# Routing search in six rounds of 7 and 5 x 5 bits beside the experts, with packed count products

## The chip, the cores and the metric

The kernel runs on one core of a Trainium2 chip. The core has TensorE (PE in the rows; PEld is its weight load), VectorE (DVE), ScalarE (ACT), GpSimd (POOL) and SyncE (SP), which work in parallel, each through its own queue in order, and wait for one another by semaphores. The metric is the time of one execution in microseconds; the profile's times are counted from the span's start.

## The reference

A recurrent attention makes 3072 rows x of 384 numbers, a router with capacity sends each row to one of eight experts, and a shared two-layer network follows:

```python
f = 1.0 / (1.0 + np.exp(-f_logit))
for t in range(S):
    state = f[:, :, t, :, None] * state + np.einsum('bhd,bhe->bhde', k[:, :, t], v[:, :, t])
    y[:, :, t] = np.einsum('bhd,bhde->bhe', q[:, :, t], state)
...
logits = x @ w_gate
for idx in np.argsort(-logits.flatten()):
    tok, e = (int(idx) // E, int(idx) % E)
    if assigned[tok] >= 0 or counts[e] >= cap:        # cap = N // E = 384
        continue
    assigned[tok] = e
    counts[e] += 1
...
h = np.maximum(x[mask] @ w1[e], 0.0)                  # 384 -> 1024
out[mask] = h @ w2[e]                                 # 1024 -> 384
...
h = x @ w_in                                          # 384 -> 2048
g = np.where(h > 0.0, h, np.exp(np.minimum(h, 0.0)) - 1.0)
g @ w_out                                             # 2048 -> 384
```

## The kernel before

**Stages.** `attention` runs to about 135 us of the span. Then `route_and_feed` finds the first expert that fills up and its 384 rows, and from about 174 us it runs eight experts, one after the other, 0 to 7. While TensorE computes expert k, VectorE searches the rows of expert k+1.

**An expert.** Each weight matrix and each activation is split in a high and a low part, and a product is three matmuls: high by high, low weight by high, high weight by low. A block is nine matmuls with 384 columns. The order of blocks on TensorE is written out in `order()`: eight "h" (first layer, `hidden`), each feeding a "y" (second layer, `output`); the last two y blocks are done column by column ("y_end" 0 to 2, `output_end`, six matmuls each); then "g01" (gates 0 and 1 together) and "g" 2 to 15 (`gated`), each followed some blocks later by its "o" (`back`). The last three o blocks of an expert stand between the next expert's first h blocks. ScalarE reads each gate from PSUM (L1177, L1178, L1181) and makes the high part t_hi (L1169), GpSimd makes `whole` (L1109) and the low part t_lo (L1081), and the o block waits for t_lo (L1449). At the end of y, ScalarE copies y_hi (L1193) and VectorE subtracts y_lo (L1522). The last thing in `output_end` is a wait of TensorE for its own last product (`y_done`), after which it raises `used`.

**The search.** For each expert to come, the threshold is found digit by digit. A round is: VectorE computes the limits of all values of the digit (L1588), compares the 24 tiles of `best` with them (L1548; `compare_first`, L100, for the first digit) into `slot_hot`; TensorE counts by products with `held` (a "visit", L1289, or L1285 where two tiles of 64 limits stand side by side in one product and VectorE adds the halves by L1596); VectorE compares the counts with the room (L1597 or L1599); TensorE sums the result (a visit, L1294); VectorE reads the digit (L1601) and adds it to `prefix` (L1607). Digits are 7, 7, 6, 6, 6 bits beside experts (7, 5, 5, 5, 5, 5 for the first search, which runs alone). Four visits follow: sums by `held_over` (L1299, whose input comes by L1613 to L1619), ties (L1301), offsets (L1304) and the list (L1315). `order()` holds a table that says behind which block each visit stands: one for expert 0 (`start`), one for experts 1 to 5, one for expert 6 (`last`). TensorE works in order, so a visit whose input isn't there holds everything behind it. The y_lo of the running expert stand in VectorE's row between two steps of the search (`visits_before_y`).

**Behind the search.** `begin(k + 2)` makes the next `best`, `compare_halves` does the first comparison of the search after next's start (two L100 of 1536 elements), and then VectorE makes w_low of the next expert's weights (L1533), x_lo (L1527) and the rest of w_low (L1539). Ahead of the first w_low it waits for `rows_asked`, which GpSimd raises behind the last of three gathers of the next rows (L1061); these stand in GpSimd's row between its steps on gates 7 to 9 (9 to 11 in expert 0). The gathered rows are turned by TensorE (`turn_x`, L1347) in three steps behind o blocks, all through the same bank r_ps; step m waits for x_lo of step m - 1.

**Expert 0.** GpSimd also makes w_out_low there, two (L1092) behind each t_lo of an h.

## Time and profile before

| | us |
|---|---|
| median of 3 runs | 852.0 (851.53 to 852.79) |
| profiled execution, time | 847.2 |
| its span | 845.5 |
| TensorE busy in the span | 784.0 (93%) |
| VectorE | 497.0 (59%) |
| ScalarE | 465.1 (55%) |
| GpSimd | 524.9 (62%) |

TensorE ends the chain that ended last with 81% of it. A busy share is a mean over stages: the attention to 135 us, the first search to 174 us, and eight experts, of which those from 263.7 us on take 78 to 83 us each. The matmuls are pipelined: a duration of 0.34 us with the next one starting 0.176 us later is TensorE at its full rate, so what an expert loses is read from the starts.

### The profile page before, as it was taken

How to read it: one execution, taken by the hardware profiler on the slowest of the kernel's cores; microseconds unless marked ns; L12 is line 12 of the kernel's file. 1: busy time of each engine (PE TensorE's matmuls, PEld its weight loads, DVE VectorE, ACT ScalarE, POOL GpSimd, SP SyncE). 2: the span in 40 equal slices, each digit the busy share in tenths (PEclk: the TensorE clock that was granted, in tenths of full speed). 3: DMA queues.
4: the chain of work that ended last, by engine and by line, in shares of the span. 5: the costliest groups of instructions: out<-in, count | busy, mean ns of one | idle time of the engine just before them, and what ended most of it. 6: DMA issues, size and time to landing. Idle time of an engine off the chain costs nothing.

```text
span 845.5 us, 17776 instructions
## 1 busy us (share of the span) xinstructions
PE 784.0 (93%) x6078; PEld 743.5 (88%) x6078; DVE 497.0 (59%) x1035; ACT 465.1 (55%) x980; POOL 524.9 (62%) x500
## 2 busy tenths in 40 slices
PE   3999995488989999999999999999999999999995
PEld 2888884487989999999999999999999999999995
DVE  6899988884695567457645863586457516430001
ACT  5677766141674277427742864287337734753653
POOL 8788883467775368537852775287518754954552
PEclk9999997598999999999999999999999999999998
DMA  6777691400130041004100410040004004100000
GB/s 195 209 210 208 191 366 45 174 14 1 60 115 6 29 150 29 2 28 150 29 5 26 151 29 16 14 160 19 29 2 159 20 29 150 29 1 29 2 1 29
DMA packets 33740, 65.70 MB, mean 78 GB/s; under 512 B 4560, under 2 KB 20944, under 8 KB 33280
## 3 DMA queue, kind: packets, MB, share of 16 engines
q1 hardware_dynamic: 27072, 50.36, 18.1%
q0 software_dynamic: 3136, 9.64, 3.5%
q10 hardware_dynamic: 3456, 4.72, 1.6%
q8 instruction: 44, 0.72, 0.3%
q14 instruction: 32, 0.26, 0.1%
HBM read 55.26 MB, written 9.44 MB: 77 GB/s over the span
## 4 chain that ended last, share of the span: by engine, by line
PE 81%; POOL 6%; issue 4%; DVE 3%; ACT 3%; DMA 2%; SPq 0%; ACTq 0%; POOLq 0%; DVEq 0%
PE o_ps L1449 8%; PE o_ps L1450 8%; PE o_ps L1451 8%; PE m_ps L1437 7%; PE m_ps L1438 6%; PE m_ps L1433 6%; PE m_ps L1374 4%; PE m_ps L1375 4%; PE m_ps L1372 4%; PE a_ps L637 3%; PE o_ps L1392 3%; PE y_ps L604 3%; PE o_ps L1394 3%; PE o_ps L1393 3%; PE xr_ps L580 2%
## 5 line engine op out<-in xcount | busy, mean ns | idle before, releaser
L1081 POOL TENSOR_TENSOR t_lo<-whole,t_hi 128x384 fp32r<-128x384 f32 x190 | 202.5, 1067 | 93.9 <-ACT t_hi L1162 92.0
L1109 POOL TENSOR_TENSOR whole<-whole,below 128x384 f32<-128x384 f32 x126 | 135.3, 1074 | 156.9 <-ACT below L1181 156.1
L1437 PE MATMUL m_ps<-y_hi,w_in_hi 128*128 128x384 f32 x384 | 134.7, 351 | 3.7 <-PE o_ps L1409 2.8
L1449 PE MATMUL o_ps<-w_out_hi,t_hi 128*128 128x384 f32 x378 | 129.1, 341 | 4.3 <-POOL t_lo L1081 3.7
L1438 PE MATMUL m_ps<-y_hi,w_in_low 128*128 128x384 f32 x384 | 130.0, 338 | 0.0
L1450 PE MATMUL o_ps<-w_out_low,t_hi 128*128 128x384 f32 x378 | 128.0, 339 | 0.0
L1451 PE MATMUL o_ps<-w_out_hi,t_lo 128*128 128x384 f32 x378 | 127.9, 338 | 0.0
L1177 ACT ACTIVATE whole<-m_ps 128x384 f32<-128x384 f32 x128 | 62.6, 489 | 90.0 <-PE m_ps L1433 82.9
L1161 ACT ACTIVATE whole<-m_ps 128x384 f32<-128x384 f32 x64 | 31.4, 491 | 124.5 <-PE m_ps L1372 111.0
L1433 PE MATMUL m_ps<-y_lo,w_in_hi 128*128 128x384 f32 x384 | 86.9, 338 | 0.0
L1449 PEld LDWEIGHTS o_ps<-w_out_hi,t_hi 128*128 128x128 f32 x378 | 71.0, 188 | 8.2 <-issue 8.2
L1437 PEld LDWEIGHTS m_ps<-y_hi,w_in_hi 128*128 128x128 f32 x384 | 72.3, 188 | 5.8 <-issue 5.8
L1181 ACT ACTIVATE below<-below 128x384 f32<-128x384 f32 x128 | 67.2, 525 | 16.8 <-ACT below L1178 0.8
L1169 ACT CAST t_hi<-whole 128x384 fp32r<-128x384 f32 x128 | 64.0, 500 | 15.4 <-POOL whole L1109 14.3
L1438 PEld LDWEIGHTS m_ps<-y_hi,w_in_low 128*128 128x128 f32 x384 | 72.3, 188 | 0.0
L1450 PEld LDWEIGHTS o_ps<-w_out_low,t_hi 128*128 128x128 f32 x378 | 71.0, 188 | 0.0
L1451 PEld LDWEIGHTS o_ps<-w_out_hi,t_lo 128*128 128x128 f32 x378 | 70.9, 188 | 0.0
L1433 PEld LDWEIGHTS m_ps<-y_lo,w_in_hi 128*128 128x128 f32 x384 | 69.2, 188 | 0.0
L1374 PE MATMUL m_ps<-x_hi,w_hi 128*128 128x384 f32 x192 | 66.4, 346 | 0.3 <-ACT x_hi L1211 0.3
L1375 PE MATMUL m_ps<-x_hi,w_low 128*128 128x384 f32 x192 | 64.7, 337 | 0.0
L1178 ACT ACTIVATE below<-m_ps 128x384 f32<-128x384 f32 x128 | 62.1, 485 | 0.0
L1548 DVE TENSOR_TENSOR slot_hot<-best,r_ps 128x1536 bf16<-128x1536 f32 (+1 forms) x24 | 51.7, 2154 | 2.6
(250 smaller groups left out, 1698.8 us busy)
## 6 DMA issues: line engine op xcount, KB each, us to landing
w_raw<-w SPq DMA_DIRECT2D x16, 1536.0 KB, 6.6
f_in<-f_t SPq DMA_DIRECT2D x48, 96.0 KB, 2.4
k_in<-k_t SPq DMA_DIRECT2D x48, 96.0 KB, 2.4
q_in<-q_t SPq DMA_DIRECT2D x48, 96.0 KB, 2.3
v_in<-v_rows SPq DMA_DIRECT2D x24, 192.0 KB, 2.8
x_scratch<-x_row ACTq DMA_DIRECT2D x24, 192.0 KB, 2.5
w_in_raw<-w_in SPq DMA_DIRECT2D x1, 3072.0 KB, 10.9
w_out_raw<-w_out SPq DMA_DIRECT2D x1, 3072.0 KB, 21.0
```

Source lines behind the costliest of these rows:

```text
L1081: nc.gpsimd.tensor_tensor(t_lo[n % RING][:], whole[n % 3][:], t_hi[n % RING][:], ALU.subtract).then_inc(lo_made, 1)
L1109: nc.gpsimd.tensor_tensor(tile[:], tile[:], below[m % 2][:], ALU.subtract).then_inc(g_made, 1)
L1169: nc.scalar.copy(t_hi[n % RING][:], whole[n % 3][:]).then_inc(g_upper, 1)
L1181: nc.scalar.activation(below[m % 2][:], below[m % 2][:], ACT.Relu, bias=1.0, scale=-1.0).then_inc(below_ready, 1)
L1374: nc.tensor.matmul(m_ps[m % RING][:], w1_hi[:, t, cols], x_hi[:, t, :], start=(t == 0), stop=False)
L1375: nc.tensor.matmul(m_ps[m % RING][:], w1_low[:, t, cols], x_hi[:, t, :], start=False, stop=False)
L1433: ins = nc.tensor.matmul(bank[:], w_in_hi[:, t, cols], y_lo[:, t, :], start=False, stop=(t == KD - 1))
L1437: nc.tensor.matmul(bank[:], w_in_hi[:, t, cols], y_hi[:, t, :], start=(t == 0), stop=False)
L1438: nc.tensor.matmul(bank[:], w_in_low[:, t, cols], y_hi[:, t, :], start=False, stop=False)
L1449: nc.tensor.matmul(o_ps[t][:], hi[:, rows], w_out_hi[:, m, :], start=(m == 0), stop=False)
L1450: nc.tensor.matmul(o_ps[t][:], hi[:, rows], w_out_low[:, m, :], start=False, stop=False)
L1451: ins = nc.tensor.matmul(o_ps[t][:], lo[:, rows], w_out_hi[:, m, :], start=False, stop=(m == MI - 1))
```

## The change

The one set of digits is now 7, 5, 5, 5, 5, 5 bits for every search. In the searches beside experts, the rounds of 5 bits compare 24 x 32 elements, write them densely, and one product counts four tiles of 32 limits (`reach_quad`, six products of 32 columns); VectorE adds the four parts by three chained subtracts from the room. A search has thus twelve visits for its digits where it had ten, and the tables of `order()` for expert 0 and for experts 1 to 5 are new. `compare_halves` first copies `best` to PSUM (`best_ps`, in the bank r_ps) and compares from there; `turn_x` therefore waits for that comparison. VectorE's wait ahead of w_low is now for `lo_made`, t_lo 9 of the running expert (11 in expert 0, 5 in expert 6). `output_end` no longer waits for its last product; the first gated product raises `used` instead. `gated` does all high parts first and then the low parts gate by gate, with the high-part products of gates 0 and 1 as before. Four of the nine tables that VectorE makes at the end of the attention are gone.

```diff
-DIGITS = [7, 7, 6, 6, 6]
-DIGITS_FIRST = [7, 5, 5, 5, 5, 5]
+DIGITS = [7, 5, 5, 5, 5, 5]
...
-                for name, digits in (("ways", DIGITS), ("ways_first", DIGITS_FIRST)):
-                    for i in range(1, len(digits)):
-                        wide = consts[name].shape[2]
...
+                for i in range(1, len(DIGITS)):
...
+    def packed(r, i):
+
+        return not is_first(r) and i > 0
...
+        quads_hot = slot_hot[:].rearrange("p t w -> p (t w)")[:, 0:tiles * QUARTER].rearrange("p (t w) -> p t w", w=QUARTER)
...
+        best_ps = r_ps[:, 512 - tiles:512]
+        reach_quad = r_ps[:, 80:80 + 4 * experts]
...
             elif start:
-                visits = {("h", 3): 0, ("h", 4): 1, ("y", 2): 2, ("h", 6): 3, ("h", 7): 4, ("y", 4): 5, ("y_end", 0): 6, ("y_end", 2): 7,
-                          ("g", 2): 8, ("g", 3): 9, ("o", 1): 10, ("o", 2): 11, ("o", 3): 12, ("o", 5): 13}
+                visits = {("h", 3): 0, ("h", 4): 1, ("h", 5): 2, ("y", 2): 3, ("y", 3): 4, ("h", 7): 5, ("y", 5): 6, ("y_end", 0): 7,
+                          ("g01", 0): 8, ("g", 2): 9, ("g", 4): 10, ("o", 0): 11, ("o", 1): 12, ("o", 2): 13, ("o", 3): 14, ("o", 5): 15}
             else:
-                visits = {("h", 0): 0, ("h", 1): 1, ("y", 0): 2, ("h", 4): 3, ("h", 5): 4, ("y", 2): 5, ("y", 3): 6, ("h", 7): 7,
-                          ("y", 5): 8, ("y_end", 0): 9, ("g01", 0): 10, ("g", 3): 11, ("o", 0): 12, ("o", 2): 13}
+                visits = {("h", 0): 0, ("o", MI - 2): 1, ("h", 2): 2, ("h", 3): 3, ("h", 4): 4, ("y", 1): 5, ("y", 2): 6, ("h", 6): 7,
+                          ("h", 7): 8, ("y", 4): 9, ("y_end", 0): 10, ("y_end", 2): 11, ("g01", 0): 12, ("g", 3): 13, ("o", 0): 14, ("o", 2): 15}
...
             def turn_x(k, m, bank):
                 if m == 0:
+                    if k + 1 < experts - 1:
+                        pe.wait_ge(hit_ready, marks_till(k + 1, 2))
...
-                if j == KD - 1:
-                    pe.wait_ge(y_done, k * KD + KD)
-                    pe.sem_inc(used, 1)
...
+                        if low:
+                            continue
                         for m in tiles_of:
                             bank, cols = m_ps[(MH + m) % RING], slice(m * P, (m + 1) * P)
...
+                            ins = nc.tensor.matmul(bank[:], w_in_hi[:, t, cols], y_hi[:, t, :], start=(t == 0), stop=False)
+                            if t == 0 and m == 0:
+
+                                ins.then_inc(used, 1)
+                            nc.tensor.matmul(bank[:], w_in_low[:, t, cols], y_hi[:, t, :], start=False, stop=False)
+                for m in tiles_of:
+                    bank, cols = m_ps[(MH + m) % RING], slice(m * P, (m + 1) * P)
+                    for t in range(KD):
+                        ins = nc.tensor.matmul(bank[:], w_in_hi[:, t, cols], y_lo[:, t, :], start=False, stop=(t == KD - 1))
+                    ins.then_inc(mm_done, 1)
...
             def compare_halves():
+                then(v.tensor_copy(best_ps, best[:]))
                 for half in range(2):
-                    compare_first(v, consts, scan, slice(half * tiles // 2, (half + 1) * tiles // 2)).then_inc(hit_ready, 1)
+                    compare_first(v, consts, scan, slice(half * tiles // 2, (half + 1) * tiles // 2), best_ps).then_inc(hit_ready, 1)
...
+                        for part in range(1, 4):
+                            rows = slice(part * QUARTER, (part + 1) * QUARTER)
+                            then(v.tensor_tensor(room_left[:], rem[rows] if part == 1 else room_left[:],
+                                                 reach_quad[rows, part * experts:(part + 1) * experts], ALU.subtract))
+                        v.tensor_tensor(reached_by[5][0:wide], reach_quad[0:wide, 0:experts], room_left[0:wide], ALU.is_ge).then_inc(hit_ready, 1)
...
-                dve.wait_ge(rows_asked, k + 2)
+                dve.wait_ge(lo_made, k * NT + MH + (12 if start else 6 if last else 10))
```

VectorE, a later round of the search beside expert 0. Before:

```order
L1588 TENSOR_SCALAR r_ps<-ways,prefix,order_mask 128x64
L1548 TENSOR_TENSOR slot_hot<-best,r_ps 128x1536
L1596 TENSOR_TENSOR room_left<-rem,r_ps 64x8
L1597 TENSOR_TENSOR reached_6<-r_ps,room_left 63x8
L1601 TENSOR_REDUCE digit<-r_ps 128x1
```

And now (the line numbers of the changed kernel differ by a few):

```order
L1589 TENSOR_SCALAR r_ps<-ways,prefix,order_mask 128x32
L1548 TENSOR_TENSOR slot_hot<-best,r_ps 128x768
L1599 TENSOR_TENSOR room_left<-rem,r_ps 32x8
L1599 TENSOR_TENSOR room_left<-room_left,r_ps 32x8 x2
L1601 TENSOR_TENSOR reached_5<-r_ps,room_left 31x8
L1605 TENSOR_REDUCE digit<-r_ps 128x1
```

The comparison has half the elements, and three subtracts stand where one stood.

TensorE in expert 1, from the last output product to the first gated one (`o_ps2` is the third block of y, `m_ps0` and `m_ps1` are gates 0 and 1). Before:

```order
L1407 MATMUL o_ps2<-t_hi3,w2_hi 128x384
L1408 MATMUL o_ps2<-t_hi3,w2_low_2402 128x384
L1409 MATMUL o_ps2<-t_lo3,w2_hi 128x384
L1437 MATMUL m_ps0<-y_hi,w_in_hi 128x384
L1438 MATMUL m_ps0<-y_hi,w_in_low_49 128x384
```

And now:

```order
L1404 MATMUL o_ps2<-t_hi3,w2_hi 128x384
L1405 MATMUL o_ps2<-t_hi3,w2_low_2398 128x384
L1406 MATMUL o_ps2<-t_lo3,w2_hi 128x384
L1289 MATMUL r_ps<-reached_5,ones 128x8
L1429 MATMUL m_ps0<-y_hi,w_in_hi 128x384
```

The last digit's visit moved here, from between the first and the second third of the output end.

TensorE in expert 0, from the output of gate 0 to gate 5, where a digit's visit now stands. Before:

```order
L1449 MATMUL o_ps2<-w_out_hi,t_hi0 128x384
L1450 MATMUL o_ps2<-w_out_low_50,t_hi0 128x384
L1451 MATMUL o_ps2<-w_out_hi,t_lo0 128x384
L1437 MATMUL m_ps1<-y_hi,w_in_hi 128x384
L1438 MATMUL m_ps1<-y_hi,w_in_low_49 128x384
```

And now:

```order
L1449 MATMUL o_ps2<-w_out_hi,t_hi0 128x384
L1450 MATMUL o_ps2<-w_out_low_50,t_hi0 128x384
L1451 MATMUL o_ps2<-w_out_hi,t_lo0 128x384
L1289 MATMUL r_ps<-reached_5,ones 128x8
L1429 MATMUL m_ps1<-y_hi,w_in_hi 128x384
```

This is the last digit of that search; before, it stood two blocks earlier, behind gate 3. The sums visit that needs it stands behind the output of gate 1 in both.

## Rows read from the trace of the kernel before

**Rows 1.** Stretches: length, busy us (and count) of PE, PEld, DVE, ACT, POOL; clock, DMA.

```profile
203.00:206.00 3.00, 2.63 (x19) 2.36 (x20) 0.88 (x3) 0.48 (x1) 2.14 (x3) 0.50 0.00 0
...
264.00:347.00 83.00, 81.84 (x548) 78.49 (x548) 51.44 (x100) 45.59 (x96) 48.37 (x47) 1.00 0.15 54
```

**Rows 2.** Waits of TensorE, 174 to 846 us: total, times, longest.

```profile
PE o_ps L1449 <- POOL t_lo L1081: 3.7, 7, 0.9
PE m_ps L1437 <- PE o_ps L1409: 2.8, 6, 0.5
PE r_ps L1347 <- DMA x_rows<-x_scratch,ids: 2.4, 1, 2.4
```

**Rows 3.** Order of time, TensorE, a visit in expert 2: start, us, instruction.

```profile
364.01 0.46 PE L1285 MATMUL r_ps<-held,slot_hot 128*128 128x16 bf16 x12
364.33 0.42 PE L1392 MATMUL o_ps<-t_hi,w_hi 128*128 128x384 f32 x1
364.59 0.34 PE L1393 MATMUL o_ps<-t_hi,w_low 128*128 128x384 f32 x1
```

**Rows 4.** VectorE's groups by line, 174 to 760 us: busy, mean ns.

```profile
L1548 DVE TENSOR_TENSOR slot_hot<-best,r_ps 128x3072 bf16<-128x3072 f32 x6 | 20.1, 3354 | 0.7
...
L1596 DVE TENSOR_TENSOR room_left<-rem,r_ps 64x8 f32<-64x8 f32 x18 | 3.0, 165 | 19.9 <-PE r_ps L1285 19.9
```

**Rows 5.** Order of time, VectorE, a round of the search in expert 2.

```profile
366.24 0.17 DVE L1601 TENSOR_REDUCE digit<-r_ps 128x1 int32<-128x8 f32 x1 [1.38 <-PE r_ps L1294]
...
367.15 1.75 DVE L1548 TENSOR_TENSOR slot_hot<-best,r_ps 128x1536 bf16<-128x1536 f32 x1
369.76 0.16 DVE L1596 TENSOR_TENSOR room_left<-rem,r_ps 64x8 f32<-64x8 f32 x1 [0.86 <-PE r_ps L1285]
369.96 0.16 DVE L1597 TENSOR_TENSOR reached<-r_ps,room_left 63x8 bf16<-63x8 f32 x1
```

**Rows 6.** Order of time, VectorE, towards the sums, in expert 0 and 2.

```profile
217.35 0.97 DVE L1613 TENSOR_TENSOR line<-prefix,order_mask 128x1 int32<-128x1 int32 x1
...
221.18 1.43 DVE L1619 TENSOR_TENSOR held_over<-held,over_line 128x384 bf16<-128x384 bf16 x1
...
377.39 0.55 DVE L1619 TENSOR_TENSOR held_over<-held,over_line 128x384 bf16<-128x384 bf16 x1
```

**Rows 7.** Order of time, TensorE in expert 2: first gate, first output block.

```profile
378.83 0.41 PE L1437 MATMUL m_ps<-y_hi,w_in_hi 128*128 128x384 f32 x1 [0.45 <-PE o_ps L1409]
...
386.64 0.68 PE L1433 MATMUL m_ps<-y_lo,w_in_hi 128*128 128x384 f32 x3
387.47 0.41 PE L1449 MATMUL o_ps<-w_out_hi,t_hi 128*128 128x384 f32 x1
```

**Rows 8.** Order of time, VectorE and GpSimd around the third gather.

```profile
408.62 4.96 DVE L1533 TENSOR_TENSOR w_low<-w_raw,w_hi 128x1024 fp32r<-128x1024 f32 x3
...
409.36 2.01 POOL L1081 TENSOR_TENSOR t_lo<-whole,t_hi 128x384 fp32r<-128x384 f32 x1
411.51 1.84 POOL L1061 DMA_INDIRECT x_rows<-x_scratch,ids  x1
...
414.43 1.00 POOL L1081 TENSOR_TENSOR t_lo<-whole,t_hi 128x384 fp32r<-128x384 f32 x1
```

**Rows 9.** The chain that ended last, in order of time: start, us.

```profile
127.58 0.54 DVE ways L465 x4
```

**Rows 10.** Order of time, VectorE, GpSimd and TensorE in expert 0.

```profile
176.94 4.25 DVE L100 TENSOR_TENSOR slot_hot<-best,limit 128x1536 bf16<-128x1536 f32 x2
...
179.53 4.61 POOL L1092 TENSOR_TENSOR w_out_low<-w_out_raw,w_out_hi 128x384 fp32r<-128x384 f32 x2
...
203.37 0.66 PE L1407 MATMUL o_ps<-t_hi,w_hi 128*128 128x384 f32 x1 [2.10 <-POOL t_lo L1081]
```

**Rows 11.** Order of time, VectorE and TensorE at the end of expert 0.

```profile
249.47 5.08 DVE L1533 TENSOR_TENSOR w_low<-w_raw,w_hi 128x1024 fp32r<-128x1024 f32 x3
...
254.72 0.52 PE L1347 MATMUL r_ps<-ident,x_rows 128*128 128x128 f32 x3 [2.36 <-DMA x_rows<-x_scratch,ids]
```

More of the change, by code:

```diff
@@ L873, in route_and_feed @@
         rem, own, open_tok = consts["rem"], consts["own"], consts["open_tok"]
-        reached_by = {bits: sb(f"reached_{bits}", [P, experts], BF16) for bits in (5, 6, 7)}
+        reached_by = {bits: sb(f"reached_{bits}", [P, experts], BF16) for bits in (5, 7)}
         digit = sb("digit", [P, 1], I32)
@@ L1267, in visit @@
             def visit(r, n, last=False):
-                rounds = 0 if last else rounds_of(r)
+                rounds = 0 if last else ROUNDS
                 at = n - 2 * rounds
@@ L1277, in visit @@
                         for half in range(2):
-                            if half == 0 and not (n == 0 or is_first(r)):
+                            if half == 0 and not is_first(r):
                                 pe.wait_ge(hit_ready, marks_till(r, 3 * i + 2))
@@ L1282, in visit @@
                             pe.sem_inc(pe_turn, 1)
[L1283 to L1286 removed]
+                            if packed(r, i):
+                                for t in (range(middle, tiles, 4) if half else range(0, middle, 4)):
+                                    ins = nc.tensor.matmul(reach_quad, quads_hot[:, t:t + 4].rearrange("p t w -> p (t w)"),
+                                                           held[:, t:t + 4].rearrange("p t e -> p (t e)"), start=(t == 0), stop=(t == tiles - 4))
                                 continue
@@ L1293, in visit @@
                         rows = slice(0, ways if ways > HALF else P)
-                        ins = nc.tensor.matmul(digit_ps, ones[rows, :], reached_by[digits_of(r)[i]][rows, :], start=True, stop=True)
+                        ins = nc.tensor.matmul(digit_ps, ones[rows, :], reached_by[DIGITS[i]][rows, :], start=True, stop=True)
                 else:
@@ L1541, in compare @@
             def compare(r, i, lim):
-                wide = ways_of(r, i) + 1
+                wide = ways_of(i) + 1
                 halves = 2 if is_first(r) else 1
@@ L1546, in compare @@
                     some = slice(half * tiles // halves, (half + 1) * tiles // halves)
-                    to = pairs_hot[:, some, 0:wide] if paired(r, i) else above[:, some, 0:wide]
+                    to = quads_hot[:, some] if packed(r, i) else above[:, some, 0:wide]
                     v.tensor_tensor(to, best[:, some].unsqueeze(2).to_broadcast(every),
@@ L1594, in search @@
                     seen()
-                    if paired(r, i):
-                        then(v.tensor_tensor(room_left[:], rem[HALF:P], reach_pair[HALF:P, experts:2 * experts], ALU.subtract))
-                        v.tensor_tensor(reached_by[6][0:wide], reach_pair[0:wide, 0:experts], room_left[0:wide], ALU.is_ge).then_inc(hit_ready, 1)
+                    if packed(r, i):
+                        for part in range(1, 4):
[3 more added lines that the diff above has]
+                        v.tensor_tensor(reached_by[5][0:wide], reach_quad[0:wide, 0:experts], room_left[0:wide], ALU.is_ge).then_inc(hit_ready, 1)
                     else:
-                        v.tensor_tensor(reached_by[digits_of(r)[i]][0:wide], reach_ps[0:wide], rem[0:wide], ALU.is_ge).then_inc(hit_ready, 1)
+                        v.tensor_tensor(reached_by[DIGITS[i]][0:wide], reach_ps[0:wide], rem[0:wide], ALU.is_ge).then_inc(hit_ready, 1)
                     seen()
```

65 lines of the change are left out of this document (24 added, 41 removed).

## Prediction

> **What bounds the kernel now.** I read the waits of TensorE first, then the table of stretches, then TensorE's order of time inside one expert, and VectorE's and GpSimd's beside it. From about 174 us on the kernel is a chain of TensorE products: in the stretch 264 to 347, one whole expert, TensorE is busy 81.84 of 83.00 us at the full 2.4 GHz [rows 1]. Here the reader is to see that only three things can shorten it: fewer instructions in TensorE's row, waits inside it, and the stage before 210 us, where the row has holes and the clock once falls. The waits that recur are short [rows 2]: seven for t_lo of GpSimd (3.7 us), six before the gated products (2.8 us), and once 2.4 us for gathered rows. VectorE (the routing search) and ScalarE are behind TensorE's row and cost nothing unless a search visit finds its input unready.
>
> **What it costs TensorE to visit the search.** Twelve small products take 364.33 - 364.01 = 0.32 us [rows 3], so 0.026 us each, and twenty-four 0.61. I take 0.026 for the 32 columns of the new ones too, 0.16 us for six (0.14 to 0.32, as if columns counted). The product behind a visit is followed after 364.59 - 364.33 = 0.26 us instead of 0.176: 0.09 us more. A digit product is 0.04. Before, one of the five searches inside experts 1 to 5 costs 0.61 x 2 + 0.32 x 3 + 0.04 x 5 + 0.09 x 10 = 3.3 us. After: 0.61 + 0.16 x 5 + 0.04 x 6 + 0.09 x 12 = 2.7 us. That is -0.55 each, **-2.75 us**. In expert 0 most of it falls into a stage that GpSimd bounds; I count nothing there.
>
> **Whether VectorE keeps up, in experts 1 to 5.** The second comparison was 3072 wide, 3.35 us, the 64-way ones 1536, 1.75 us [rows 4, 5], 1.04 ns an element beyond a fixed 0.15; 768 lie on that line at 0.95. From a count product to the digit product before: subtract, compare, semaphore: 0.17 + 0.20 + 0.17. The new form has three chained subtracts, about 0.20 start to start each (room_left at 369.76, reached at 369.96 [rows 5]), so 0.95 us behind the count, and the cover is one block of nine products, 1.58 + 0.09 us. From a digit product to the next count: digit 366.24, comparison 367.15 [rows 5], so 0.9 + 0.95 + 0.3 of semaphores = 2.1 us; the cover is two blocks, 3.2 us, or at least 2.7 in front of the first output end. Every visit has 0.6 us or more to spare: no wait. If that cover is gone, each visit costs its shortage in full, since TensorE works in order.
> The tightest is the visit behind gates 0 and 1. The last digit is read behind the three y_lo; ScalarE's y_hi (0.5) and the last y_lo (0.55) with their semaphores put that some 1.4 us behind the last output product; the chain digit to held_over takes 1.7 when GpSimd is idle (held_over 0.55, [rows 6]); the block covers 3.3 us. It just fits; 0 to 0.3 us each.
> A page of the Trainium skill speaks against this part: "VectorE: DVE Perf Modes", section "Rules for kernel authors", advises for chained operations to minimize their number. By that alone the search gets longer (rival (e)). The rows say: some seventeen small operations more are 17 x 0.20 = 3.4 us, and 7680 - 3840 = 3840 compared elements fewer at 1.04 ns are 4.0 us, so the search stays about as long.
>
> **The drain before the gates.** The removed wait holds TensorE until its last output product has left: idle 0.45 us by the row [rows 7], and 0.61 late against the free pitch of 0.176. Such gaps stand in experts 1 to 7: 0.61 five times, 0.70 and 0.77, in all 4.5 us. What is late next is y_hi of the third block: 0.5 us of ScalarE behind the product; the gate needs it only eight products on. All goes: **-4.5**, and the restart of 0.08 in 6 and 7.
>
> **The first second-layer block.** Three y_lo products start at 386.64, so that the block could start at 386.64 + 0.53 = 387.17, and it starts at 387.47 [rows 7]: 0.3 us of waiting for t_lo 0, in each of seven experts 0.2 to 0.6. The chain starts at gate 0's last product, which moves from fifth to third of six: 0.35 us earlier. I take **-2.1** (0 to -2.6).
>
> **First comparison and the later start of w_low.** At 407 to 413 GpSimd's t_lo takes 2.01 and the issue of a gather 1.84 us, against 1.00 for the t_lo at 414.43 [rows 8], while VectorE runs the first comparison (both inputs in SBUF) and then w_low. The latter was to wait for the gathers, yet it starts at 408.62, before the third at 411.51. With an input in PSUM the comparison leaves GpSimd alone, as I take from the search's own comparisons; w_low now waits for a t_lo that follows the third gather. So the output block behind gate 12, which comes 0.56 to 0.80 us late in experts 1 to 4 (four of the seven waits for t_lo [rows 2]), is on time: 2.5 us, and restarts, **-2.8**. w_low then ends near 417.8, just before x_lo asks for VectorE. The copy to PSUM, some 0.2 us, is hidden.
> Sum for experts 1 to 7: 2.75 + 4.6 + 2.1 + 2.8 = **-12.3 us**.
>
> **Up to expert 0.** Four table operations of VectorE go, 0.54 us of the chain that ends last [rows 9]: **-0.5**. At 177 to 185 GpSimd is the bound: the first comparison (4.25 for two) and w_low double its operations, two w_out_low take 4.61 for 2.0 [rows 10]. About 2.5 us of its 4 us of delay lie beside the comparison. TensorE later stands 2.10 us for the last t_lo at 203.37 [rows 10]: this and 0.4 before it shrink to about 1: **-2.5** (-1 to -3.2).
> The granted clock was 0.50 from 203 to 206 [rows 1], the level of 1.2 GHz, behind that idle time of 2.1; the eighteen products of the output end cost 0.32 instead of 0.176, 2.6 us. At 254.72 an idle time of 2.36 [rows 11] left the clock whole. With 1 us of idle I expect it not to fall: **-2.6** (0 to -2.6). The drain in front of the gates: **-0.5**.
>
> **What the change costs in expert 0.** The sums visit stands behind the output of gate 1, as before, but the last digit now comes two blocks, not four, ahead of it. The chain digit to held_over there runs beside a GpSimd that is never idle: it begins just before 217.35, each of its five steps on SBUF inputs takes about 1 us, held_over 1.43 to 222.61 [rows 6], 5.7 us in all. The cover is now 3.3 us. **+2.6** (0 to +3).
> The gather for expert 1: TensorE stands 0.9 us for t_lo [rows 2] and 2.36 us for the rows [rows 11]. Free of VectorE, GpSimd asks for the rows 2.3 us earlier. But w_low (5.08 us, [rows 11]) now starts only behind t_lo 11, about 251.5, and ends near 256.5; x_lo follows it, and the second transpose needs x_lo. So 3.2 us go and 2.5 come back: **-0.7** (-3.2 to +0.5).
> Sum to here: -0.5 - 2.5 - 2.6 - 0.5 + 2.6 - 0.7 = **-4.2 us**.
>
> **Total.** -12.3 - 4.2 = -16.5 us. The profiled execution has a span of 845.5 and a time of 847.2; it would be 830.7. The median of the runs is 852.0, 4.8 above, and I find nothing in the trace for that, so I subtract the same: **835.5 us**.
>
> **Rivals.**
> (a) Expert 0 gives nothing back: the sums chain finds GpSimd idle, or w_low is not late for x_lo. For it: GpSimd's backlog is smaller once the comparison leaves it alone. Against: the rows at 217 are of a backlog made by the gates, which stays. 835.5 - 2.6 - 2.4 = 830.5.
> (b) The clock falls all the same, at the output end or behind one of the two new waits of 2.5 us. For: 2.10 sufficed once. Against: 2.36 did not. Some 2.6 us each: 838 to 841.
> (c) The drain, t_lo and gather terms come in half, other waits replacing them: half of 9.5, 840.
> (d) Slower. The small operations of the search are not as free of GpSimd as at 369.76: GpSimd makes a t_lo in each h block, and if a subtract meets it, it takes 1.0 instead of 0.17. Three in a row then need 3.4 us where 1.67 are covered, 1.8 us for each of five visits, 9 us for a search, 45 us for five: 880. It decides from 3.3 us per expert, that is if over a third of these visits are hit. Against: eighteen subtracts of this kind, one input in PSUM, have a mean of 0.165 in this stage [rows 4].
> (e) No change: the small operations lengthen each search by 3.4 us, and the comparisons, bound by something other than their elements, don't get shorter; where TensorE waits for all of it, five times 3.4 = 17 us eat the gain: 852. Against: 3.35 and 1.75 us for 3072 and 1536 [rows 4, 5]. This is what the skill's rule on the number of operations would make of it.
> (f) The change isn't what it says: the new wait never binds, because its t_lo is always long made when VectorE arrives. Then the -2.8 shrinks to what the comparison does, about half: 837, inside the range.
>
> **Chances.** Forecast 0.52; (a) 0.15; (b) 0.13; (c) with (f) 0.14; (d) 0.03; (e) 0.03, within 0.2% (1.7 us, about what a measurement of this kernel can tell from no change). Range 830 to 843: it takes in (a), (b), (c) and the ends of the small terms. Faster 0.94, same 0.03, slower 0.03.
>
> **What the profile would show.** An expert of 80.4 instead of 82.9 us from first product to first product; the waits L1437 behind L1409 gone and those for t_lo down to two or three; the third gather's issue 1.0; w_low behind it; granted clock 1.00 at 200 to 206; a wait of TensorE for held_over near 217 and one for x_lo near 250. It is wrong if TensorE waits at the search's visits in experts 1 to 5, or if the clock falls behind the new waits.

## The result, and the profile after

The changed kernel is faster. Its median over four runs is 828.4 us (827.1 to 829.1) against 851.8 us (846.1 to 852.8) for the kernel before beside it: a ratio of 0.974 (95% interval 0.969 to 0.978). The forecast was 835.5 with a range of 830 to 843: right in sign, its range missed by 1.6 us at the low end. The two medians stand 23.4 us apart, where the forecast had 16.5. The profiled execution has a time of 829.0 and a span of 827.2, against 847.2 and 845.5: 18.3 us less, where the sum said 16.5.

TensorE's waits from 174 to 846 us, the view of [rows 2], are now all of these (total, times, longest):

```profile
PE r_ps L1344 <- DVE x_lo L1527: 1.9, 1, 1.9
PE r_ps L1294 <- DVE held_over L1623: 1.9, 1, 1.9
PE o_ps L1404 <- POOL t_lo L1076: 0.9, 1, 0.9
PE m_ps L1371 <- ACT x_hi L1206: 0.7, 1, 0.7
PE o_ps L1449 <- POOL t_lo L1076: 0.2, 1, 0.2
```

The six waits before the gates and the seven for t_lo in front of L1449 are gone but for 0.2 us; the two waits that the prediction added in expert 0, for held_over and x_lo, are there. The stretches answer to [rows 1]; the columns are the same (before the last two, the granted clock):

```profile
203.00:206.00 3.00, 3.00 (x20) 3.00 (x19) 2.73 (x6) 1.11 (x3) 0.58 (x1) 1.00 0.00 0
...
245.00:260.00 15.00, 13.06 (x69) 12.46 (x68) 9.20 (x8) 7.28 (x16) 11.17 (x9) 0.89 0.05 13
260.00:341.00 81.00, 81.00 (x523) 78.04 (x522) 49.67 (x118) 46.13 (x97) 50.67 (x47) 1.00 0.16 55
```

At 203 to 206 the clock is whole, as forecast. From 260 to 341 TensorE is busy in all of 81.00 us. At 245 to 260 the clock falls for a while, behind the wait for x_lo; the prediction had named a fall behind a new wait as one of its signs of being wrong. Expert 1 now takes 80.34 us (82.94), experts 2 to 5 80.1 to 80.4 (82.0 to 83.1). TensorE's order of time in expert 2, at the last gate ahead of the first output block (compare [rows 7]):

```profile
378.29 0.42 PE L1429 MATMUL m_ps<-y_hi,w_in_hi 128*128 128x384 f32 x1
...
379.42 0.69 PE L1437 MATMUL m_ps<-y_lo,w_in_hi 128*128 128x384 f32 x3
379.94 0.38 PE L1449 MATMUL o_ps<-w_out_hi,t_hi 128*128 128x384 f32 x1
```

The output block starts 0.52 us behind the first of three y_lo products, with no gap (0.83 before). And VectorE and GpSimd around the third gather, for [rows 8]:

```profile
397.70 3.42 DVE L100 TENSOR_TENSOR slot_hot<-r_ps,limit 128x1536 bf16<-128x1536 f32 x2
...
399.87 1.02 POOL L1104 TENSOR_TENSOR whole<-whole,below 128x384 f32<-128x384 f32 x1 [1.45 <-ACT below L1176]
400.85 1.01 POOL L1076 TENSOR_TENSOR t_lo<-whole,t_hi 128x384 fp32r<-128x384 f32 x1
402.01 1.03 POOL L1056 DMA_INDIRECT x_rows<-x_scratch,ids  x1
...
405.23 5.14 DVE L1533 TENSOR_TENSOR w_low<-w_raw,w_hi 128x1024 fp32r<-128x1024 f32 x3 [4.11 <-POOL t_lo L1076]
```

GpSimd's operations beside the comparison (it ends at 401.1) take 1.0 us; the third gather, beside a VectorE that stands, 1.03 instead of 1.84; and w_low stands 4.11 us for the new wait.

### The profile page after: what moved, and what is told of

Read it like the earlier page. It is cut to its first block, busy times and chain, and to the rows that moved or that the text cites. A ratio compares the mean times of both kernels' runs of the same rounds, so it can differ in the third digit from the quotient of the medians.

```text
span 827.2 us, 17547 instructions
## 1 busy us (share of the span) xinstructions
PE 774.5 (94%) x5904; PEld 737.3 (89%) x5904; DVE 480.5 (58%) x1138; ACT 465.8 (56%) x980; POOL 531.1 (64%) x500
## 4 chain that ended last, share of the span: by engine, by line
PE 87%; DVE 4%; POOL 3%; issue 2%; DMA 1%; ACT 1%; SPq 0%; DVEq 0%; POOLq 0%; ACTq 0%
PE o_ps L1449 8%; PE m_ps L1429 8%; PE o_ps L1451 8%; PE m_ps L1433 8%; PE m_ps L1437 8%; PE o_ps L1450 8%; PE m_ps L1371 4%; PE m_ps L1372 4%; PE m_ps L1369 4%; PE a_ps L635 3%; PE o_ps L1389 3%; PE y_ps L602 3%; PE o_ps L1391 3%; PE o_ps L1390 3%; PE xr_ps L578 2%
## 5 line engine op out<-in xcount | busy, mean ns | idle before, releaser
L1076 POOL TENSOR_TENSOR t_lo<-whole,t_hi 128x384 fp32r<-128x384 f32 x190 | 212.1, 1118 | 91.3 <-ACT t_hi L1157 89.5
L1104 POOL TENSOR_TENSOR whole<-whole,below 128x384 f32<-128x384 f32 x126 | 138.2, 1097 | 135.7 <-ACT below L1176 135.1
L1449 PE MATMUL o_ps<-w_out_hi,t_hi 128*128 128x384 f32 x378 | 130.5, 345 | 0.3 <-POOL t_lo L1076 0.2
L1450 PE MATMUL o_ps<-w_out_low,t_hi 128*128 128x384 f32 x378 | 125.6, 332 | 0.0
L1172 ACT ACTIVATE whole<-m_ps 128x384 f32<-128x384 f32 x128 | 62.8, 490 | 84.9 <-PE m_ps L1437 83.4
L1176 ACT ACTIVATE below<-below 128x384 f32<-128x384 f32 x128 | 67.4, 527 | 16.8 <-ACT below L1173 0.8
L1449 PEld LDWEIGHTS o_ps<-w_out_hi,t_hi 128*128 128x128 f32 x378 | 71.1, 188 | 1.4 <-issue 1.1
L1533 DVE TENSOR_TENSOR w_low<-w_raw,w_hi 128x1024 fp32r<-128x1024 f32 x24 | 41.1, 1768 | 36.4 <-POOL t_lo L1076 36.3
```

Source lines behind the costliest of these rows:

```text
L1076: nc.gpsimd.tensor_tensor(t_lo[n % RING][:], whole[n % 3][:], t_hi[n % RING][:], ALU.subtract).then_inc(lo_made, 1)
L1104: nc.gpsimd.tensor_tensor(tile[:], tile[:], below[m % 2][:], ALU.subtract).then_inc(g_made, 1)
L1176: nc.scalar.activation(below[m % 2][:], below[m % 2][:], ACT.Relu, bias=1.0, scale=-1.0).then_inc(below_ready, 1)
L1449: nc.tensor.matmul(o_ps[t][:], hi[:, rows], w_out_hi[:, m, :], start=(m == 0), stop=False)
L1450: nc.tensor.matmul(o_ps[t][:], hi[:, rows], w_out_low[:, m, :], start=False, stop=False)
```

## The experiments

Spans cannot be compared term by term, because expert 0 and the first stage differ from execution to execution (below). What repeats is the time from the first product of expert 1 to the last product of all ("experts 1 to 7"): it is 572.5 and 572.3 us in two traces of the kernel before, 557.4 and 557.5 in two of the changed one. The table gives it for each kernel, and beside it expert 0 and the start of expert 0's first product, all from the starts of products in the traces.

| kernel | expert 0 starts | expert 0 | experts 1 to 7 |
|---|---|---|---|
| before | 174.3 | 89.4 | 572.5 |
| before, again | 174.3 | 88.6 | 572.3 |
| before, 32 bytes | 174.0 | 89.6 | 571.8 |
| before, 224 bytes | 174.9 | 90.7 | 571.1 |
| before, drain removed | 173.4 | 90.7 | 565.0 |
| before, comparison from PSUM | 178.9 | 83.3 | 569.4 |
| the same, w_low later | 179.3 | 84.1 | 569.5 |
| digits alone | 179.1 | 91.8 | 567.8 |
| changed | 174.0 | 86.4 | 557.4 |
| changed, again | 177.3 | 86.0 | 557.5 |
| changed, 32 bytes | 174.2 | 85.5 | 559.0 |
| changed, two numbers of expert 0 | 175.0 | 83.3 | 557.3 |
| changed, throwaway products | 173.5 | 84.9 | 557.3 |
| all of these | 173.4 | 80.3 | 558.0 |

**The kernel before once more.** No edit.

> The kernel before, unchanged, once more. Its runs without a profile took 851.5 to 852.8 us and one 846.1, its profiled run 847.2; the changed kernel's four runs lie within 2 us (827.1 to 829.1), and its profiled run among them. Theory 1: this kernel has two ways to go, one about 5 us longer, that differ by whether the granted clock falls behind waits in expert 0 or before it; then the runs here fall into two groups, near 847 and near 852, and the mean granted clock goes with them (0.973 in the shorter). Theory 2: profiling itself shortens this kernel by 5 us; then every run without a profile is 851 to 853 and the profiled one 847. Theory 3: the first measurement drifted; then all are alike, 846 to 848 or 851 to 853.

Measured: twelve runs from 845.2 to 852.6, median 849.2; the runs of the kernel before in the same comparison 844.1 to 853.2, median 847.4 (25 runs), and in the next, on another chip, 852.3 (10 runs). So theory 2 falls, since many runs without a profile are as short as the profiled one, and theory 3 too. Theory 1 is borne out in part. The mean granted clock goes with the time of these twelve runs: it is 0.974 to 0.976 in the six up to 848.6 us and 0.970 to 0.972 in the six from 849.9 on. By an estimate from these numbers, 0.004 of 847 us is 3.4 us of full rate lost, most of the distance. Where the clock falls is not fixed: in this trace it does not fall at 203 to 206 (it was 0.50 in [rows 1]) but at 253.7, and the time is within 1 us of the first profile. And it isn't all: in the comparison with the median of 852.3, runs of 846.8, 847.2, 852.3 and 852.4 us all have a mean clock of 0.973. The 4.8 us that the prediction carried from the profile to the median were the chance of three runs.

**Where the spread comes from.** Comparing traces from the start, the long ones part from the short ones at 22 us, in the attention. TensorE's order of time, first the kernel before (again), then the kernel before with the comparison from PSUM:

```profile
21.79 1.16 PE L637 MATMUL a_ps<-q_s,k_s 48*128 48x128 f32 x16
22.88 1.15 PE L580 MATMUL xr_ps<-turn_gate,x_tr 112*128 112x120 f32 x8
23.96 1.08 PE L594 MATMUL y_ps<-q_s,state 48*48 48x128 f32 x16
```

```profile
21.83 2.08 PE L638 MATMUL a_ps<-q_s,k_s 48*128 48x128 f32 x16
23.84 2.06 PE L581 MATMUL xr_ps<-turn_gate,x_tr 112*128 112x120 f32 x8
25.83 1.95 PE L595 MATMUL y_ps<-q_s,state 48*48 48x128 f32 x16
27.71 1.95 PE L605 MATMUL y_ps<-a_m,v_in 128*48 128x128 f32 x16
```

The same sixteen products take 1.16 or 2.08 us: until about 30 us TensorE runs at half its rate there, and expert 0 starts 4 to 5 us later. The granted clock of the stretches 22 to 28 us is written as 1.00 in both traces, but no record stands behind it: the traces hold no record of the clock before 21.6 us and before 31.2 us, and the view counts time without a record as full. Where the record begins is where the products speed up. Three more traces (later w_low, digits alone, the changed kernel again) are of the late kind, and the changed kernel has it too. No trace of the kernel before, unedited, is of the late kind. Of the experiments, the four traces of the comparison with the median of 847.4 are all early, three of the four of that with 852.3 are late; each comparison had a chip of its own, so the chip may set the share, which was not tested.

> The changed kernel, unchanged, once more. In the traces so far the products of TensorE in the first stage (a_ps, xr_ps, y_ps at 22 to 29 us) follow each other every 103 to 112 ns in some executions and every 207 to 214 ns in others, until about 29 us, whatever the kernel; all that follows is then some 4 us later. Theory S: this, and not the profiling, is the spread of 847 and 852 of the kernel before, and the changed kernel has it too: its runs fall into a group at 827 to 829 and one at 831 to 833, in other shares than in the first four. Rival: the changed kernel does not have it, all runs at 827 to 829.

Measured: 827.1, 828.2, 831.0, 832.0, 833.8, 833.8, median 831.5, against 848.3 (11 runs) for the kernel before: ratio 0.980 (0.976 to 0.983). Its trace has the late rise:

```profile
22.34 2.08 PE L635 MATMUL a_ps<-q_s,k_s 48*128 48x128 f32 x16
...
177.25 0.66 PE L1371 MATMUL m_ps<-x_hi,w_hi 128*128 128x384 f32 x1 [0.32 <-ACT x_hi L1206]
```

Theory S is right in that the late rise is there in the changed kernel and costs it 3.2 us ahead of expert 0 (177.25 for 174.01). It is not all of the spread: the two runs of 833.8 have the lowest mean clocks of the six (0.971 and 0.972), so falls later on add to it. That the first four runs of the changed kernel were short and three of the first four of the kernel before long follows from their times alone; by which of the two sources those three were long is not shown. The difference of the medians was 23.4 us then and 16.8 here. To test what sets the moment, products were added where TensorE stood still ahead of it:

```diff
+            def warm(products):
+                for _ in range(products):
+                    nc.tensor.matmul(xr_ps[:, 0, :], ident[:], ident[:], start=True, stop=True)
...
+                    if isinstance(s, int) and s == 3:
+                        warm(3)
                     scores(pb, c, s == 3)
+                    if isinstance(s, int) and s == 3:
+                        warm(8)
```

> The changed kernel with eleven throwaway products of TensorE (ident by ident into a bank that is not yet in use) added in the first stage, three in front of and eight behind the first a_ps products at 14.6 us, where TensorE otherwise stands still until 18.4. Theory S: with TensorE at work there, the rate rises before 21.8 us in every execution; no run of 831 or more is left, and the median is 826.5 to 828.5. Rival: the moment of the rise does not depend on this work; the same two groups as the changed kernel in this comparison.

Measured in the same comparison as the changed kernel again: six runs from 823.1 to 827.9, median 825.7, against 831.5. No run reaches 831, where four of the six of the changed kernel do, and the median is below the forecast. Of the 5.1 us between the two profiled runs, 3.8 lie ahead of expert 0 (it starts at 173.5 for 177.25) and 1.1 in it. The last experiment has the same products and shows the rise:

```profile
17.33 3.78 PE L642 MATMUL xr_ps<-ident 128*128 128x128 f32 x16
21.04 1.09 PE L602 MATMUL y_ps<-a_m,v_in 128*48 128x128 f32 x16
```

With TensorE at work from 13.9 to 21.0 us, its products go at the full rate from 21.04 on. Both traces with these products have the early rise, but so have eight of the twelve without; it is the run times that speak for theory S. The spread left, 4.8 us, goes largely with the mean granted clock, 0.978 in the shortest run and 0.974 in the longest; that the falls behind the waits of expert 0 make it is likely (the spread is 2.6 with two of those waits shortened or gone, below), not shown.

**Where the tensors lie.** The gated products, which no edit was meant to touch, follow each other faster: start to start 172.9 ns against 176.4, nine in 1.56 us against 1.58. Smaller tables for the digits and one small tile less had moved y_hi and all that is reserved behind it, from byte 199648 of a partition to 197568. Three kernels have unused bytes reserved in front of `digit`, 32 of them as here, or 224 by a width of 56:

```diff
+        spare = sb("spare", [P, 8], I32)
         digit = sb("digit", [P, 1], I32)
```

> The kernel before with 32 unused bytes per partition reserved behind the search's tables, so that y_hi, y_lo, x_hi, x_lo, t_hi, t_lo and the per-expert weights lie at multiples of 64 bytes, as in the changed kernel, and not 32 beyond. No instruction differs. Theory L (place in SBUF): the nine products of a gated tile take 1.56 us instead of 1.58 (172.9 instead of 176.4 ns each), 1152 products in all, some 2.5 to 3.5 us faster than before. Rival (order): the pitch of the gated products came from the changed order of the products, or from the missing drain; then nothing changes, 0.0 +- 0.5 us.

> The changed kernel with the same 32 unused bytes, which bring y_hi and the rest to 32 bytes beyond a multiple of 64, as in the kernel before. Theory L: gated products at 176.4 ns again, 2.5 to 3.5 us slower than the changed kernel (831 to 832). Rival: nothing changes, 828 to 829.

> The kernel before with 224 unused bytes per partition reserved instead of 32, so that y_hi lies at 199872, which has the same remainder by 256 as in the changed kernel (197568), where 32 bytes brought it to one by 64 alone and left the gated products at 175.9 ns. If the remainder by 256 decides, the gated products take 172.9 ns and each of experts 1 to 5 is 0.2 to 0.4 us shorter (82.4 to 82.6 for 82.7 to 82.8); if a larger distance or the order of the products decides, they stay near 176.

Measured, as y_hi's remainder by 256, the mean distance of gated products, and that of the o products:

| kernel | remainder | gated, ns | o, ns |
|---|---|---|---|
| before; changed with 32 bytes; drain removed | 224 | 176.4 | 175.5 |
| before with 32 bytes | 0 | 175.9 | 176.0 |
| changed; digits alone; throwaway products | 192 | 172.9 to 173.0 | 175.9 to 176.0 |
| before with 224 bytes | 192 | 172.9 | 175.8 |

One such block in the changed kernel, and with 32 bytes, by the start of its first product and of the next block's:

```profile
399.42 0.33 PE L1429 MATMUL m_ps<-y_hi,w_in_hi 128*128 128x384 f32 x1
...
400.98 0.35 PE L1449 MATMUL o_ps<-w_out_hi,t_hi 128*128 128x384 f32 x1
```

```profile
395.67 0.34 PE L1430 MATMUL m_ps<-y_hi,w_in_hi 128*128 128x384 f32 x1
...
397.25 0.34 PE L1450 MATMUL o_ps<-w_out_hi,t_hi 128*128 128x384 f32 x1
```

So the place decides, not the order of the products or the drain: the kernel before with 224 bytes has its old order and the new pace (one trace), and with the drain removed the new order has the old pace. The remainder by 64 does not suffice (0 in the second row), that by 256 orders the three that were tried. It is a rule of three points and no more; which operand it goes by stays open. In time it is small: 572.3 - 571.1 = 1.2 us one way, 559.0 - 557.4 = 1.6 the other. The gated products alone give 3.0 us in both pairs. In the kernel before 1.2 of that comes back in front of the output blocks behind them, which wait for t_lo ten times and 4.1 us from 264 us on, for seven times and 2.9 us in the kernel before again; in the changed kernel these starts and slower o products take 1.0 together. The expected 2.5 to 3.5 us, and 0.2 to 0.4 for each expert, were too many (with 224 bytes experts 2 to 5 are 0.15 to 0.23 us shorter and expert 1 is 0.04 longer), and the medians (848.1 for 847.4; 830.5) cannot show it.

**The drain.** The three lines of the wait in `output_end` are gone, and `gated` is that of the changed kernel.

```diff
-                if j == KD - 1:
-                    pe.wait_ge(y_done, k * KD + KD)
-                    pe.sem_inc(used, 1)
```

> The kernel before, with only the wait of TensorE for its last second-layer product removed, and the three low products of each of gates 0 and 1 issued together behind the high ones (gate 0 done first). Forecast in the prediction: 4.5 for the wait, 0.5 for expert 0, and up to 2.1 for the first output of the second layer, whose t_lo starts 0.35 us earlier: 4.5 to 7 us faster. Rival, if ScalarE's y_hi is late next: half, 2.5 to 3.5. The gated pitch stays at 176.4 ns by theory L.

Measured: 839.2 us (eight runs, 837.2 to 845.1) for 847.4, ratio 0.992 (0.988 to 0.995); experts 1 to 7 take 572.3 - 565.0 = 7.3 us less, 0.6 above the forecast of 4.6 + 2.1. The seven steps from y to the first gate give 4.4, the steps from gates to output blocks 2.1, and a restart of 0.07 us behind each of the seven drains 0.5, where the prediction counted it in two. In expert 2:

```profile
377.13 0.34 PE L1409 MATMUL o_ps<-t_lo,w_hi 128*128 128x384 f32 x1
377.31 0.34 PE L1432 MATMUL m_ps<-y_hi,w_in_hi 128*128 128x384 f32 x1
```

From 0.61 us late [rows 7] to the plain distance of 0.18. Not all waits for t_lo are gone by it: four remain, 1.9 us together, those of the other cause.

**The comparison from PSUM, and w_low later.** The first with the lines of the change in `compare_first`, `compare_halves`, `turn_x` and the first visit; the second also

```diff
-                dve.wait_ge(rows_asked, k + 2)
+                dve.wait_ge(lo_made, k * NT + MH + (12 if start else 6 if last else 10))
```

> The kernel before, with only the first comparison of each search reading best from a copy in PSUM (with the two waits of TensorE that this needs). Theory P (two SBUF inputs of VectorE hold up GpSimd, one in PSUM does not): GpSimd's operations beside the comparison take 1.0 us and not 1.9 to 2.0. From the first product of expert 0 to its first gated product 33.3 to 33.4 us become about 31 (before, where the clock does not fall; 35.6 where it falls). The t_lo waits of experts 1 to 4 (2.5 us in all) shrink by half, since w_low still starts beside the gathers. In all 3.5 to 4.5 us faster, and fewer runs near 852. Rival R (the delay is not the comparison's but w_low's alone): GpSimd as slow as before beside the comparison, nothing gained. Rival N (the PSUM form does nothing for the time of the comparison but adds a copy on the chain): +0.2 us per search.

> As the kernel with the comparison from PSUM, and VectorE's w_low waits for a t_lo behind the third gather. Theory P: the t_lo waits of experts 1 to 4 are gone altogether, 2.5 to 2.8 us for experts 1 to 7 in the two changes together, and the third gather's issue takes 1.0 us everywhere; in expert 0 the x_lo of the next expert is waited for, 1.9 to 3.7 us, and the granted clock falls behind it (so up to 2 us of the gain goes there). Rival (w_low was never early enough to matter): the same time and the same waits as with the comparison from PSUM alone.

Measured: 841.5 (840.1 to 843.0) and 843.5 (838.6 to 844.4) for 852.3; ratios 0.987 (0.985 to 0.990) and 0.989 (0.985 to 0.992). With the comparison alone, beside it at 181.8 (VectorE 3.42 us for two):

```profile
182.16 1.02 POOL L1083 TENSOR_TENSOR t_lo<-whole,t_hi 128x384 fp32r<-128x384 f32 x1 [4.67 <-ACT t_hi L1164]
183.13 2.00 POOL L1094 TENSOR_TENSOR w_out_low<-w_out_raw,w_out_hi 128x384 fp32r<-128x384 f32 x2
185.09 1.00 POOL L1083 TENSOR_TENSOR t_lo<-whole,t_hi 128x384 fp32r<-128x384 f32 x1
186.05 3.82 POOL L1094 TENSOR_TENSOR w_out_low<-w_out_raw,w_out_hi 128x384 fp32r<-128x384 f32 x2
```

Two w_out_low take 2.00 beside the comparison and 3.82 beside w_low that follows it: theory P. The comparison itself is no faster: 1752 ns against 1755. The Trainium skill, "SBUF — State Buffer", section "SBUF: two separate sides", says that a VectorE operation with two SBUF inputs and one of GpSimd that reads SBUF exclude each other; these rows agree. From the first product of expert 0 to its first gated product it is 30.5 us for 33.4 (forecast about 31). Expert 0 as a whole goes from 88.6 to 83.3 us, part of it because the clock, which fell at 253.7 in the kernel before again, does not fall here. Experts 1 to 7 give 572.3 - 569.4 = 2.9, all that was forecast for the comparison and the later w_low together. That makes 8.2 us in the traces where 3.5 to 4.5 were expected. With w_low later, experts 1 to 7 are the same (569.5), and TensorE's waits for t_lo from 264 us on are 1.0 us, in three, with and without it; so the rival of the second expectation holds. In expert 0 x_lo is waited for 1.4 us (1.9 to 3.7 expected) and the clock does not fall behind it. With the comparison alone, the third gather beside an early w_low in expert 2 takes 1.83 us, and TensorE does not feel it:

```profile
407.43 1.83 POOL L1063 DMA_INDIRECT x_rows<-x_scratch,ids  x1 [0.15 <-issue]
```

So the later w_low, a wait that binds for 4.11 us, is worth nothing here, and my theory P was wrong in its half for it.

**The digits alone.** The changed kernel with the three other parts undone.

> The changed kernel with the other parts undone: only digits of 7, 5, 5, 5, 5, 5 bits, four tiles a product, and the visits as in the changed kernel. Forecast in the prediction: each of experts 1 to 5 0.55 us shorter than before (82.8 becomes 82.2), tables -0.5, and a wait for held_over of some 2 us in expert 0: in all 1 to 3 us faster. Rival, if VectorE does not keep up: r_ps <- room_left or reached waits in experts 1 to 5 and experts of 83 us or more. Gated products at 176.4 or at 172.9 ns: the addresses are those of the changed kernel, so 172.9 if the place in SBUF decides alone, and 2.5 to 3 us more of gain, 176.4 if the missing drain has to do with it.

Measured: 845.9 (843.1 to 849.7) for 852.3, ratio 0.993 (0.990 to 0.997). Experts 1 to 7: 572.3 - 567.8 = 4.5, of which 1.2 to 1.6 are the place in SBUF (173.0 ns here): 3.1 for five searches, 0.6 each where 0.55 was forecast. The medians stand 6.4 us apart, more than the 1 to 3 expected. VectorE's groups of 264 to 760 us:

```profile
L1542 DVE TENSOR_TENSOR slot_hot<-best,r_ps 128x768 bf16<-128x768 f32 x25 | 23.9, 955 | 2.7
...
L1592 DVE TENSOR_TENSOR room_left<-room_left,r_ps 32x8 f32<-32x8 f32 x50 | 8.0, 160 | 1.7
```

The 768 wide comparison takes 955 ns (forecast 0.95 us) and fifty chained subtracts 160 ns each (the longest of all 75 subtracts is 164 ns): none met GpSimd, and TensorE has no wait for room_left or reached. Rivals (d) and (e) had no ground. Expert 0 is 3.2 us longer than in the kernel before again, 2.1 of it the wait for held_over.

**Two numbers of expert 0.** Where the visits of the sums and behind them stand, and behind which t_lo w_low starts:

```diff
-                          ("g01", 0): 8, ("g", 2): 9, ("g", 4): 10, ("o", 0): 11, ("o", 1): 12, ("o", 2): 13, ("o", 3): 14, ("o", 5): 15}
+                          ("g01", 0): 8, ("g", 2): 9, ("g", 4): 10, ("o", 0): 11, ("g", 6): 12, ("g", 7): 13, ("g", 8): 14, ("o", 5): 15}
...
-                dve.wait_ge(lo_made, k * NT + MH + (12 if start else 6 if last else 10))
+                dve.wait_ge(lo_made, k * NT + MH + (11 if start else 6 if last else 10))
```

> The changed kernel with two numbers of expert 0 altered: the visit for the sums one gated block later (and the next two visits each one block earlier than their output block), and w_low of VectorE after the eleventh t_lo of the gated tiles, not the twelfth. Theory: both new waits of TensorE, 1.9 us for held_over near 218 and 1.9 us for x_lo near 251, go or shrink below 0.3, and with the second the fall of the granted clock at 253 (1.4 us): 3.5 to 5 us faster than the changed kernel, 824 to 825. Rival (the waits only move: the x_rows or the first x_hi are late next, and the clock falls all the same): 0 to 2 us faster.

Measured: 828.8 (826.8 to 831.4), ratio 0.974 (0.972 to 0.976) to a kernel before at 852.3: the changed kernel, 828.4 and 831.5 in two other comparisons, was not in this one, so the runs show neither the 3.5 to 5 us expected nor their absence. The trace: expert 0 at 83.3 for 86.4 us, of which 1.1 lie ahead of its first gated product, where nothing was edited (the clock is 1.00 at 172 to 178 for 0.50); held_over's wait 0.4 for 1.9, the clock 1.00 at 245 to 260, but

```profile
PE r_ps L1344 <- DVE x_lo L1527: 1.8, 1, 1.8
...
PE r_ps L1344 <- DMA x_rows<-x_scratch,ids: 1.1, 1, 1.1
```

The wait for x_lo did not go: x_lo stood behind three w_low that now began earlier and ran longer (244.4 to 252.2 for 247.7 to 252.8). Half right.

**All of these.** The throwaway products, the visits above, the gathers one gated tile earlier, w_low behind the tenth t_lo, and the first x_lo ahead of w_low:

```diff
-                lower_first(k + 1)
-                for m in range(KD):
-                    x_lower_part(k + 1, m, r_ps)
-                    lower_second(k + 1, m)
+                if start:
+                    x_lower_part(k + 1, 0, r_ps)
+                    lower_first(k + 1)
+                    x_lower_part(k + 1, 1, r_ps)
...
-                gather_at = 9 if start else 3 if last else 7
+                gather_at = 8 if start else 3 if last else 7
```

> The changed kernel with the throwaway products, and in expert 0: the visit for the sums one gated block later (the next two one block earlier than their output blocks), the gathers for expert 1 one gated tile earlier, w_low from the tenth gated t_lo on, and the first x_lo of expert 1 ahead of the three w_low and not behind them. Theory: the waits for held_over (1.9), x_lo (1.9), the rows (1.1 in the kernel with two numbers altered) and the fall of the clock behind them (1.5) go, 4 to 6 us less than the changed kernel with throwaway products: 821 to 824. Rival: GpSimd, which bounds the start of expert 0, gives the waits back as later t_lo: 825 to 827.

Measured, in the comparison with the two kernels above: five runs from 820.5 to 823.1, median 822.8, against 825.7 with the throwaway products alone, 831.5 for the changed kernel and 848.3 for the one before; ratio to the last 0.969 (0.966 to 0.972). TensorE's waits of 174 to 262 us:

```profile
PE o_ps L1413 <- POOL t_lo L1085: 1.8, 1, 1.8
PE m_ps L1380 <- ACT x_hi L1215: 0.6, 1, 0.6
PE r_ps L1303 <- DVE held_over L1632: 0.4, 1, 0.4
```

The waits for x_lo and for the rows are gone, expert 0 takes 80.3 us. By the medians the edits of expert 0 are worth 2.9, less than the 4 to 6 expected; in the traces 84.9 - 80.3 = 4.6, of which expert 1 gives 0.7 back (80.96 for 80.22).

## Why the prediction was wrong in its range, and which of its steps held

**What bounds the kernel, the drain, VectorE keeping up.** Right. TensorE's row decides; from 264 us on the changed kernel waits for 0.2 us in all, and at no visit of the search.

**Experts 1 to 7: -12.3 said, -14.9 to -15.1 measured.** The parts, from the experiments against 572.3: digits -4.5, of which the place in SBUF is -1.2 to -1.6 (not in the sum at all) and the visits about -3.1 (said -2.75); drain and first output block -7.3 (said 4.6 + 2.1 = 6.7); comparison from PSUM -2.9 with w_low later 0 (said -2.8 for both). They add to -14.7 and leave next to nothing over. Rival (f) said that the new wait would never bind; it binds, and it was still worth nothing, which costs the forecast nothing because the comparison alone gave the whole term.

**Up to expert 0 and in it: -4.2 said, -3.3 measured** in the profiled pair (expert 0 starts 0.3 earlier and is 3.0 shorter). The tables were to give 0.5; the start is 0.3 earlier in this pair, but the kernel before and its edits with the early rise start expert 0 anywhere from 173.4 to 174.9 with all nine tables, so no run shows this term. The start of expert 0 to its first gated product is shorter by 35.56 - 30.58 = 4.98 (said 2.5 + 2.6 + 0.5 = 5.6). The sums cost 1.9 (said 2.6). What is left for the rows and x_lo is a cost of 0.07 where -0.7 was said: the wait for x_lo came out at 1.94 (said 2.5), and the clock fell behind it, which the prediction gave to rival (b) and not to the forecast. But the 2.6 for the clock at 203 were not the change's to give: the kernel before, again, does not lose them there, and loses at 245 to 262 instead (clock 0.90), and the changed kernel, again, does lose the clock at 205.6, behind a wait of 1.83 us. In pairs of single traces such a term is a chance.

**Total.** -16.5 said for the profiled pair, -18.3 measured: experts 1 to 7 gave 2.8 more than said (the place in SBUF 1.2 to 1.6, the drain 0.6, the rest the visits and a difference of 0.2 between the two traces of before), expert 0 and what is ahead of it 0.9 less.

**The step that failed** is the last: "The median of the runs is 852.0, 4.8 above, and I find nothing in the trace for that, so I subtract the same: 835.5". The 4.8 us were three long runs beside a short profile. Runs of the same kernel then went from 844.1 to 853.2 us, and the four runs of the changed kernel were short ones. Without the offset the forecast is 830.7 and its range 825 to 838, with 828.4 inside; the two medians of the changed kernel, 828.4 and 831.5, stand on either side of 830.7. That 830.7 comes so near is in part luck, since the misses of experts 1 to 7 and of expert 0 point opposite ways and one gain, the place in SBUF, was not foreseen. The range should have taken in both starting points.

## What to carry to other kernels

When the profiled execution stands away from the median of a few runs, first get more runs of the kernel before, look whether the mean granted clock goes with the time, and compare two of its traces from their start on: the difference has a place, and it may have nothing to do with the change. Freeing a second engine by moving one operand to PSUM was worth 2.9 us here in experts 1 to 7, and a wait that reorders the two nothing. A change that frees some bytes moves every tensor behind them, so keep the addresses the same where a few tenths of a per cent are to be ascribed to an edit.

## What the runs showed of the hardware

- TensorE's full rate in the first stage begins at 21 to 23 us or at 28 to 31 us, by execution, at 3 to 5 us of cost. The granted clock's column is at 1.00 in both, because the clock's record begins only at that moment (21.1 to 23.3 us, or 28.1 to 31.4). With eleven products in the gaps ahead of it both traces have the early start, and none of the eleven runs of those two kernels is above 827.9 us. The Trainium skill, "TensorE: Matmul & The Clock Gate", section "Part 1: The HAM clock gate (the "warmup" mystery)", says that the moment of the rise varies from run to run and costs under 1% of a kernel; the 4 us are 0.5% here, and as much as a term of the sum.
- Whether the clock falls behind a wait is a chance as well. In the fourteen traces, from 190 to 264 us, TensorE stands still for 3.75 us three times, and the clock falls each time; for 2.1 us five times, and it falls each time; for 2.36 to 2.41 us three times, and it falls once; for 1.65 to 1.94 us fifteen times, and it falls four times; for 1.07 to 1.44 us three times, and it never falls. At one and the same place it fell behind 1.94 us for x_lo in the changed kernel (0.89 at 245 to 260) and not behind 1.84 with the throwaway products (1.00 at 245 to 262).
- The pace of fp32 products with 384 columns varied from 172.9 to 176.4 ns with the place of their operands in SBUF alone, moved by 32 or 224 bytes.
- The issue of a gather on GpSimd takes 1.03 us beside a VectorE that stands, and 1.83 beside w_low, which reads both inputs from SBUF.
